# Attention, routed experts and feed-forward on one core: logits' units respaced, buffers moved by 160 bytes, a longer last filler

## The chip, the cores and the metric

The kernel runs on one core of a Trainium2 chip. The metric is the device time of one execution in microseconds (us). A profile of one execution by the hardware profiler shows what each engine did: TensorE (PE, its weight loads apart as PEld), VectorE (DVE), ScalarE (ACT), GpSimd (POOL) and SyncE (SP, which here only issues DMAs).

## The reference

Three blocks in a row, all in float32. Attention: 4 batches x 8 heads, 576 tokens, head size 64; scores below the row's maximum minus `tau` are masked out before the softmax. The result is rearranged to 2304 tokens x 512 features. Then a mixture of 8 experts: each token goes to the expert with the largest cosine similarity (the logits), through `relu(x @ w1[e]) @ w2[e]`, weighted by the softmax probability of that expert. Then a gated feed-forward with 1536 hidden features.

```python
    scores = np.where(scores >= thresh, scores, -1000000000.0)
    ...
    logits = xn @ en.T / tau
    expert_idx = np.argmax(logits, axis=1)
    ...
        h = np.maximum(x[mask] @ w1[e], 0.0)
        out[mask] = gate_w[mask, None] * (h @ w2[e])
    ...
    g = x @ w_gate
    silu = g * (1.0 / (1.0 + np.exp(-g)))
    val = x @ w_val
    return (silu * val @ w_out).astype(np.float32)
```

## The kernel before

Large products are made from operands split in two fp32r parts, `hi` and `lo`, with three matmuls in place of one.

**Attention** (`attention`, L166) works on 16 pairs of heads with 9 score tiles each, 144 steps, numbered g = 0 to 143. A step of TensorE is a turn of one loop (from L390): values of the step two back (`values`, L354, ten 128x66 matmuls in the trace, where the program has five float32 ones), scores of the step two ahead (`scores_tile`, L311), transposes of this step's probabilities (`probs_t`, L335). Between scores and transposes VectorE takes the maximum (L545), ScalarE the exponential (L416), VectorE the mask (`prob`, L557); after the transposes ScalarE copies them out of PSUM (`prob_t`, L423). Three PSUM buffers go round for scores and transposes, two for the values.

**Logits' units.** The logits of tokens whose heads are all done are computed among the attention steps. A unit takes some (token tile, feature chunk) blocks: `tokens_t` (L343) transposes them from `x_sb` in place of a step's probabilities, ScalarE copies them out, `logits` (L371) multiplies them with the expert embeddings (128x8 matmuls), ScalarE copies the sums out (`logits_out`, L441). A unit has its own place in the list UNITS, which sets the order on TensorE, ScalarE and VectorE: `unit_order` (L143) puts it behind the step that the table `logit_units` (L126) names. A unit has no scores, so in the turn two ahead of it TensorE has none to compute. Tiles 0 to 8 need heads of the first eight pairs (`s_x` at 8, counted by GpSimd's `normalise`, L662), tiles 9 to 17 those of the second eight; the latter are summed in parts (`part`) and added at the end by VectorE (L634 to L638).

**Experts** (`experts`, L783): after a routing stage, tokens are gathered slot by slot (128 rows, L102), transposed (`rows_t`, L908), multiplied with w1 (`hidden`, L916, L927: hp) and w2 (`output`, L943, L954: yp). Stationary operands are slices of `xt` and `ht`, moving operands are 512 columns of the weights. `keep_warm` (L959) issues matmuls whose result nobody reads, at three places of the routing stage; both operands are taken from the start of the same weight chunk. WARM (L780) has their numbers.

**Feed-forward** (`feed_forward`, L1210): 6 groups of 384 tokens by 12 chunks of 128 hidden features, 72 steps. A step has 24 matmuls of 384 columns (`gate_value`, L1331: gp and vp, stationary the weights, moving `f_xt`) and 9 of 512 columns (`add_out`, L1345: op, stationary `st`, moving the weights).

**Buffers.** The weights, `x_sb` and what lies beside them are placed from the top of SBUF downwards (`Weights`). The other buffers are placed upwards from the bottom, in the order of the code; those of the three stages begin behind `norm` (in `build`, L1489) and take each other's place. 

Of the kernel before, what the change touches and what calls it, by code (L numbers as in the profile page):

```python
# [7 lines left out]
F32 = mybir.dt.float32  # L8
F32R = mybir.dt.float32r
I32 = mybir.dt.int32  # L10
ALU = mybir.AluOpType
# [11 lines left out]
KC = FEAT // 128  # L23
# [89 lines left out]
TILES = 9  # L113
# [8 lines left out]
STEP, LOGITS = "step", "logits"  # L122
# [3 lines left out]
def logit_units():  # L126

    units = [(((t, t + 1), range(KC)), (10 + t // 3, 1 + 3 * (t % 3))) for t in range(TILES)]  # L130
    units += [(((TILES + 2 * n, min(TILES + 2 * n + 2, 2 * TILES)), range(0, 2)), (13 + n // 3, 1 + 3 * (n % 3)))
              for n in range(5)]
    thirds = ((0, 4), (4, 8), (8, 9))
    units += [(((TILES + a, TILES + b), range(2, 3)), (15, 1 + 3 * n)) for n, (a, b) in enumerate(thirds)]
    units += [(((TILES + a, TILES + b), range(3, 4)), None) for a, b in ((0, 4), (5, 9), (4, 5))]
    return units


LOGIT_UNITS = logit_units()
HEADS_4_5 = TILES + 7  # L140


def unit_order():  # L143

    behind = {at: n for n, (_, at) in enumerate(LOGIT_UNITS) if at}
    order = []
    for g in range(STEPS):
        order.append((STEP, g))
        if (g // TILES, g % TILES) in behind:
            order.append((LOGITS, behind[g // TILES, g % TILES]))  # L150
    return order + [(LOGITS, n) for n, (_, at) in enumerate(LOGIT_UNITS) if not at]


UNITS = unit_order()
UNIT_OF = {what: u for u, what in enumerate(UNITS)}

# [9 lines left out]
def attention(nc, q, k, v, tau, emb, moe_tau, w1, w2, x_rows, ys_dram, weights, ident, consts, logit,  # L166
# [7 lines left out]
    with ExitStack() as ctx:  # L174
        def sb(name, shape, dt=F32):
            return ctx.enter_context(nc.sbuf_tensor(name, shape, dt))

        def sem(name):
            return ctx.enter_context(nc.semaphore(name))
# [23 lines left out]
        part = sb("part", [128, 3, TILES, EXPERTS])  # L203
# [39 lines left out]
        s_part = sem("s_part")  # L243
# [167 lines left out]
        def _(act):  # L411
# [29 lines left out]
            def logits_out(u, n):  # L441
                (first, end), chunks = LOGIT_UNITS[n][0]
                act.wait_ge(s_o, u + 1)
                if first < TILES:
                    dst = logit[:, first:end, :]
                else:
                    dst = part[:, max(0, chunks[-1] - 1), first - TILES:end - TILES, :]
                nc.scalar.activation(dst.rearrange("p t e -> p (t e)"), o_ps[u % 2][:, 0:EXPERTS * (end - first)],
                                     ACT.Copy).then_inc(s_o_sb, 1)

# [55 lines left out]
            for u in range(len(UNITS) + 1):  # L506
                if u < len(UNITS):
                    what, g = UNITS[u]
# [5 lines left out]
                if u + 2 < len(UNITS):  # L514
                    what, g = UNITS[u + 2]
                    if what == STEP:
                        exp_tile(u + 2, g)
                if u >= 1:
                    what, g = UNITS[u - 1]
                    if what == STEP and g < LAST:  # L520
                        values_out(u - 1, g)
                    elif what == STEP:
                        last_values_out(u - 1, g)
                    else:
                        logits_out(u - 1, g)
                if u < len(UNITS) and UNITS[u][0] == STEP:
                    p, t = UNITS[u][1] // TILES, UNITS[u][1] % TILES
# [11 lines left out]
        def _(dve):  # L539
            V = nc.vector  # L540
# [29 lines left out]
            def last_sum_inv(g):  # L570
                t, u = g - LAST, UNIT_OF[STEP, g]
                dve.wait_ge(s_o, behind(g))
                if t == 0:
                    dve.wait_ge(s_x, PAIRS - 2)
                if t < 8:
                    last = V.tensor_scalar(row_sum[:, 1, t:t + 1], o_ps[u % 2][:, D:D + 1], 1e-9, None, ALU.add)
                else:
                    for side in range(2):
                        rows = slice(TAIL * side, TAIL * (side + 1))
                        last = V.tensor_scalar(row_sum[rows, 1, t:t + 1],  # L580
                                               o_ps[u % 2][rows, V_COLS * side + D:V_COLS * side + D + 1],
                                               1e-9, None, ALU.add)
                last.then_inc(s_last_inv, 1)
                dve.wait_ge(s_last_inv, 2 * t + 1)
                V.reciprocal(row_inv[:, 1, t:t + 1], row_sum[:, 1, t:t + 1]).then_inc(s_last_inv, 1)
# [36 lines left out]
            for u in range(behind(STEPS - 1) + 2):  # L622
                what, g = UNITS[u + 1]
                if what == STEP:
                    max_tile(u + 1, g)
                what, g = UNITS[u]
# [4 lines left out]
                what, g = UNITS[u - 2]  # L631
                if u >= 2 and what == STEP and g >= LAST:
                    last_sum_inv(g)
            dve.wait_ge(s_o_sb, UNIT_OF[LOGITS, HEADS_4_5] + 1)  # L634
            V.tensor_tensor(part[:, 0, :, :], part[:, 0, :, :], part[:, 1, :, :], ALU.add).then_inc(s_part, 1)
            dve.wait_ge(s_part, 1)
            dve.wait_ge(s_o_sb, len(UNITS))
            V.tensor_tensor(logit[:, TILES:2 * TILES, :], part[:, 0, :, :], part[:, 2, :, :], ALU.add)  # L638
# [138 lines left out]
        self.inv = ctx.enter_context(nc.psum_tensor("inv", [128, 2, SLOTS], F32))  # L777


WARM = (6, 20, 14)  # L780


def experts(nc, slot_rows, ys_dram, w1, w2, wg, wv, wo, weights, slot_tab, ident, logit, best, norm, squares, gate,  # L783
# [5 lines left out]
    with ExitStack() as ctx:  # L789
# [117 lines left out]
        def _(pe):  # L907
            def rows_t(i, buf, arrived):  # L908
                pe.wait_ge(s_x[buf], arrived)

                for c in range(KC):
                    last = nc.tensor.transpose(xb[:, 128 * c:128 * (c + 1)], x_in[:, buf, 128 * c:128 * (c + 1)],
                                               ident[:])
                last.then_inc(s_xt, 1)
# [44 lines left out]
            def keep_warm(n):  # L959
                w = weights.ring[0][:, 0, 0, :]  # L960
                for _ in range(n):
                    nc.tensor.matmul(yp[:], w[:, 0:128], w[:, 0:PSUM_BANK], start=True, stop=True)

            keep_warm(WARM[0])
            pe.wait_ge(s_pad, 1)
# [5 lines left out]
            last.then_inc(s_rank, 1)  # L971
            keep_warm(WARM[1])
            pe.wait_ge(s_row, 1)
            for t in range(T):
                last = nc.tensor.matmul(r.inv[:], r.row_b[:, t, :], r.token_b[:, t, :, :], start=(t == 0), stop=(t == T - 1))
            last.then_inc(s_inv, 1)
            keep_warm(WARM[2])
            rows_t(0, 0, 16)
# [493 lines left out]
def spread(a, n=128):  # L1472
    return a.rearrange("(a b) -> a b", a=1).broadcast_to([n, 1])


def build(nc, q, k, v, tau, emb, moe_tau, w1, w2, w_gate, w_val, w_out, out):
    x_rows = nc.dram_tensor("x_rows", (TOKENS, FEAT), F32, kind="Internal").ap()
    ys = nc.dram_tensor("ys", (SLOTS * 128, FEAT), F32, kind="Internal").ap()
    with ExitStack() as ctx:
        ident = ctx.enter_context(nc.sbuf_tensor("ident", [128, 128], F32))  # L1480
        pos = ctx.enter_context(nc.sbuf_tensor("pos", [128, TOK_TILES], I32))
        gate = ctx.enter_context(nc.sbuf_tensor("gate", [128, TOK_TILES], F32))
        token_of = ctx.enter_context(nc.sbuf_tensor("token_of", [128, SLOTS], I32))
        slot_tab = ctx.enter_context(nc.sbuf_tensor("slot_tab", [1, 5, SLOTS + 1], I32))
        weights = Weights(nc, ctx)
        logit = ctx.enter_context(nc.sbuf_tensor("logit", [128, TOK_TILES, EXPERTS], F32))
        best = ctx.enter_context(nc.sbuf_tensor("best", [128, TOK_TILES], F32))
        squares = ctx.enter_context(nc.sbuf_tensor("squares", [128, TOK_TILES], F32))
        norm = ctx.enter_context(nc.sbuf_tensor("norm", [128, TOK_TILES], F32))  # L1489
        s_xrows = ctx.enter_context(nc.semaphore("r_xrows"))  # L1490
        s_filled = ctx.enter_context(nc.semaphore("r_filled"))
        consts = Consts(nc, weights)
        attention(nc, q, k, v, spread(tau), emb, spread(moe_tau), w1, w2, x_rows, ys, weights, ident, consts, logit,
                  squares, s_xrows, s_filled)
        with ExitStack() as rows_ctx:
            slot_rows = SlotRows(nc, rows_ctx, x_rows, token_of)
            experts(nc, slot_rows, ys, w1, w2, w_gate, w_val, w_out, weights, slot_tab, ident, logit, best, norm, squares,
                    gate, s_filled, consts, s_xrows, pos, token_of)
        feed_forward(nc, ys, out, w_gate, w_val, w_out, weights, pos, gate, ident)
# [47 lines left out]
```

## Time and profile before

| | us |
|---|---|
| median of 3 runs | 1186.64 (1180.28 to 1188.91) |
| profiled execution | 1188.04 |
| its span, first to last instruction | 1186.1 |
| TensorE busy | 1122.5 (95%) |
| VectorE busy | 546.3 (46%) |
| ScalarE busy | 508.2 (43%) |
| GpSimd busy | 245.5 (21%) |

Attention lasts to about 393 us of the span, routing to about 412, the experts to about 687, the feed-forward to the end. The granted TensorE clock is a mean 0.982 of full speed (2.4 GHz); 0.5 is the lower of its two levels, 1.2 GHz. Matmuls are pipelined: a matmul's duration is longer than the distance to the next one's start, and a row of several (x14) lasts from the first one's start to the last one's end. In brackets stands an engine's idle time before a row, with what ended it.

### The profile page before, as it was taken

The numbers are of one execution on the slowest core, as the hardware profiler recorded it, in microseconds if no ns is written. First come the engines' busy times: TensorE is split into PE (matmuls) and PEld (weight loads), VectorE is DVE, ScalarE is ACT, GpSimd is POOL, SyncE is SP. The second block draws the span as 40 slices with busy tenths as digits, with TensorE's granted clock in tenths as the row PEclk, the third lists the DMA queues.
The fourth block names the chain that finished last, engine by engine and source line by source line (L and its number), as shares of the span: only waits on it lengthen the run. The fifth ranks groups of instructions, "written<-read, shape, count | busy, mean of one in ns | idle before, by whom it ended". The sixth has DMA issues, their size and how long they took to land. (4 is left out here: it accounts for less than half of the span.)

```text
span 1186.1 us, 19312 instructions
## 1 busy us (share of the span) xinstructions
PE 1122.5 (95%) x6837; PEld 1029.8 (87%) x6838; DVE 546.3 (46%) x910; ACT 508.2 (43%) x900; POOL 245.5 (21%) x185
## 2 busy tenths in 40 slices
PE   5999999999999799999999929999999999999996
PEld 4999999999999578888888829999999999999996
DVE  4777777765566455555433524322322323223221
ACT  4777777778676454444442423121221221212211
POOL 1433445442520101111111111212030030200000
PEclk9999999999999899999999969999999999999999
DMA  4222332341101645465424331001010010000000
GB/s 161 70 83 100 132 102 96 119 180 55 55 2 60 206 160 178 140 232 180 152 101 160 112 114 62 27 25 30 1 54 1 1 53 0 27 0 0 28 1 27
DMA packets 35687, 97.36 MB, mean 82 GB/s; under 512 B 2968, under 2 KB 5272, under 8 KB 35616
## 3 DMA queue, kind: packets, MB, share of 16 engines
q1 hardware_dynamic: 28880, 74.88, 18.1%
q0 software_dynamic: 6560, 21.50, 5.4%
q8 instruction: 46, 0.75, 0.3%
q14 instruction: 25, 0.20, 0.1%
q10 hardware_dynamic: 176, 0.02, 0.0%
HBM read 79.61 MB, written 16.78 MB: 81 GB/s over the span
## 5 line engine op out<-in xcount | busy, mean ns | idle before, releaser
L367 PE MATMUL o_ps<-v_in,prob_t 128*128 128x66 f32 (+1 forms) x1440 | 181.2, 274 | 0.2 <-ACT prob_t L423 0.2
L367 PEld LDWEIGHTS o_ps<-v_in,prob_t 128*128 128x128 f32 x1440 | 175.8, 195 | 0.4 <-ACT prob_t L423 0.4
L1440 DVE TENSOR_TENSOR act_in<-gp,sig 128x384 f32<-128x384 f32 x72 | 40.1, 557 | 277.4 <-ACT sig L1386 277.4
L545 DVE TENSOR_REDUCE neg_max<-scores 128x1 f32<-128x576 f32 x144 | 109.0, 757 | 108.5 <-PE scores L330 108.2
L1386 ACT ACTIVATE sig<-gp 128x384 f32<-128x384 f32 x72 | 35.4, 491 | 281.1 <-PE vp L1331 281.1
L423 ACT ACTIVATE prob_t<-scores 128x640 f32<-128x640 f32 (+3 forms) x164 | 112.9, 689 | 91.8 <-PE scores L340 84.9
L557 DVE SCALAR_TENSOR_TENSOR prob<-scores,thresh,expo 128x576 f32<-128x576 f32 x144 | 116.5, 809 | 3.1 <-ACT expo L416 3.1
L340 PE MATMUL scores<-ident,prob 128*128 128x128 f32 x720 | 105.8, 279 | 8.6 <-DVE prob L557 8.6
L330 PE MATMUL scores<-kt_hi,qt 128*128 128x288 f32 x320 | 104.3, 342 | 5.7 <-DVE kt_lo L617 3.0
L416 ACT ACTIVATE expo<-scores,neg_max 128x576 f32<-128x576 f32 x144 | 107.1, 744 | 4.0 <-DVE neg_max L545 4.0
L1331 PE MATMUL gp<-f_xt_hi,w_hi 128*128 128x384 f32 x288 | 99.8, 347 | 1.4 <-DVE f_xt_lo L1429 1.4
L1331 PE MATMUL gp<-f_xt_hi,w_lo 128*128 128x384 f32 x288 | 98.1, 341 | 0.0
L1331 PE MATMUL gp<-f_xt_lo,w_hi 128*128 128x384 f32 x288 | 98.1, 340 | 0.0
L1331 PE MATMUL vp<-f_xt_hi,w_hi 128*128 128x384 f32 x288 | 97.5, 339 | 0.0
L1331 PE MATMUL vp<-f_xt_lo,w_hi 128*128 128x384 f32 x288 | 97.5, 339 | 0.0
L1331 PE MATMUL vp<-f_xt_hi,w_lo 128*128 128x384 f32 x288 | 97.4, 338 | 0.0
L1304 POOL DMA_INDIRECT out<-stage,out_row x18 | 17.6, 979 | 384.3 <-ACT stage L1399 381.0
L340 PEld LDWEIGHTS scores<-ident,prob 128*128 128x128 f32 x720 | 86.7, 143 | 11.0 <-DVE prob L557 10.9
L330 PE MATMUL scores<-kt_lo,qt 128*128 128x288 f32 x320 | 91.5, 302 | 0.0
L1345 PE MATMUL op<-w_hi,st_hi 128*128 128x512 f32 x216 | 85.8, 397 | 1.7 <-DVE st_lo L1446 1.7
L1345 PE MATMUL op<-w_lo,st_hi 128*128 128x512 f32 x216 | 86.1, 398 | 0.0
L1345 PE MATMUL op<-w_hi,st_lo 128*128 128x512 f32 x216 | 85.1, 394 | 0.0
(201 smaller groups left out, 2134.4 us busy)
## 6 DMA issues: line engine op xcount, KB each, us to landing
stage<-in_moe_w SPq DMA_DIRECT2D x18, 1024.0 KB, 5.4
stage_more<-in_moe_w SPq DMA_DIRECT2D x14, 1024.0 KB, 7.6
q_raw<-in_q SPq DMA_DIRECT2D x16, 640.0 KB, 5.1
k_raw<-in_k SPq DMA_DIRECT2D x16, 576.0 KB, 3.8
ys<-y_out POOLq DMA_DIRECT2D x21, 256.0 KB, 2.3
v_in<-in_v SPq DMA_DIRECT2D x16, 330.0 KB, 2.9
stage<-in_moe_w_val SPq DMA_DIRECT2D x3, 1024.0 KB, 5.7
x_rows<-x_sb SPq DMA_DIRECT2D x1, 2304.0 KB, 9.1
```

The costliest lines, as they stand in the source:

```text
L330: last = nc.tensor.matmul(scores[u % 3][:, half, 0:HALF], qt[:, par, c:c + 128], kt[:, par, keys], start=(m == 0 and kt is kt_hi), stop=(m ...
L340: last = nc.tensor.transpose(dst[:, 128 * c:128 * (c + 1)], prob[:, g % 3, key:key + 128], ident[:])
L367: last = nc.tensor.matmul(dst, prob_t[:, u % 3, 128 * c:128 * (c + 1)], src, start=(c == 0), stop=(c == KEY_CHUNKS - 1))
L416: nc.scalar.activation(expo[:, g % 3, :].rearrange("p (a c) -> p a c", a=2), scores[u % 3][:, :, 0:HALF], ACT.Exp, bias=neg_max[:, g % TIL ...
L423: nc.scalar.activation(prob_t[:, u % 3, 0:cols], scores[u % 3][:].rearrange("p a c -> p (a c)")[:, 0:cols], ACT.Copy).then_inc(s_pt_sb, 1)
L545: V.tensor_reduce(neg_max[:, t:t + 1], scores[u % 3][:, :, 0:HALF], mybir.AxisListType.XY, ALU.max, negate=True).then_inc(s_max, 1)
L557: V.scalar_tensor_tensor(prob[:, g % 3, :].rearrange("p (a c) -> p a c", a=2), scores[u % 3][:, :, 0:HALF], thresh[:, t:t + 1], expo[:, g ...
L1304: nc.gpsimd.indirect_dma_start(out=out, out_offset=bass.IndirectOffsetOnAxis(ap=out_row[:, n:n + 1], axis=0), in_=y[:, t, :], in_offset=No ...
L1331: last = nc.tensor.matmul(dst[:, 0:GT], w[a][:, 3 * (f // 4) + which, k, 128 * (f % 4):128 * (f % 4 + 1)], xt[buf][b][:, k, :], start=(n = ...
L1345: last = nc.tensor.matmul(op[t][:], st[a][:, f % 2, 128 * t:128 * (t + 1)], w[b][:, 3 * (f // 4) + 2, f % 4, :], start=(f == 0 and n == 0) ...
L1386: nc.scalar.activation(sig[:], gp[f % 2][:, 0:GT], ACT.Sigmoid).then_inc(s_sig, 1)
L1440: nc.vector.tensor_tensor(act_in[:], gp[f % 2][:, 0:GT], sig[:], ALU.mult).then_inc(s_c, 1)
```

## The change

Four edits, shown below.

- The units get other places, and the table names the step g itself. Tiles 0 to 8 stand behind steps 79, 83, ... 111 (before: 91, 94, ... 115), four pairs of tiles with two chunks behind 116, 120, 124, 128 (before five units behind 118, 121, ... 130, the fifth with one tile). The last token tile has one unit with three chunks behind 133, and two units with four tiles follow behind 137 and 141 (before 136, 139, 142 with 4, 4 and 1 tiles). The three units behind the last step are as before. 17 units among the steps become 16; the blocks are the same 72.
- `logits_out` and VectorE's addition follow: the last tile's three chunks are summed by the unit itself, so the addition of the second part leaves that tile out.
- WARM's last number goes from 14 to 22.
- An unused buffer is placed ahead of all buffers of the three stages, so that the first of them starts a multiple of 512 bytes from the weights. In the built program it has 160 bytes: `kt_hi`, `x_in` and `rows` move from 18752 to 18912, and all that follows them moves by the same 160. `x_sb` starts at 192480.

```diff
-    units = [(((t, t + 1), range(KC)), (10 + t // 3, 1 + 3 * (t % 3))) for t in range(TILES)]
...
-    thirds = ((0, 4), (4, 8), (8, 9))
-    units += [(((TILES + a, TILES + b), range(2, 3)), (15, 1 + 3 * n)) for n, (a, b) in enumerate(thirds)]
+    units = [(((t, t + 1), range(KC)), 79 + 4 * t) for t in range(TILES)]
+    units += [(((TILES + 2 * n, TILES + 2 * n + 2), range(0, 2)), 116 + 4 * n) for n in range(4)]
+    units += [(((2 * TILES - 1, 2 * TILES), range(0, 3)), 133)]
+    units += [(((TILES + a, TILES + a + 4), range(2, 3)), 137 + a) for a in (0, 4)]
...
-HEADS_4_5 = TILES + 7
+HEADS_4_5 = TILES + 6
...
-        if (g // TILES, g % TILES) in behind:
-            order.append((LOGITS, behind[g // TILES, g % TILES]))
+        if g in behind:
+            order.append((LOGITS, behind[g]))
...
-                    dst = part[:, max(0, chunks[-1] - 1), first - TILES:end - TILES, :]
+                    dst = part[:, chunks[-1] - 1 if len(chunks) == 1 else 0, first - TILES:end - TILES, :]
...
-            V.tensor_tensor(part[:, 0, :, :], part[:, 0, :, :], part[:, 1, :, :], ALU.add).then_inc(s_part, 1)
+            rest = TILES - 1
+            V.tensor_tensor(part[:, 0, 0:rest, :], part[:, 0, 0:rest, :], part[:, 1, 0:rest, :], ALU.add).then_inc(s_part, 1)
...
-WARM = (6, 20, 14)
+WARM = (6, 20, 22)
...
+        here = -(-nc.sbuf_base // 32) * 32
+        ctx.enter_context(nc.sbuf_tensor("to_weights", [128, (weights.x_start - here) % 512 // 4], F32))
```

The order on TensorE, before, from the transposes of the second unit's tokens (`scores<-ident,x_sb`) to the values behind its logits (`o_ps<-emb_t,prob_t`); the next unit stands three tiles further:

```order
L351 MATMUL scores<-ident,x_sb 128x128 x4
L367 MATMUL o_ps<-v_in,prob_t 128x66 x5
L330 MATMUL scores<-kt_hi,qt 128x288
L330 MATMUL scores<-kt_lo,qt 128x288
L330 MATMUL scores<-kt_hi,qt 128x288
L330 MATMUL scores<-kt_lo,qt 128x288
L340 MATMUL scores<-ident,prob 128x128 x5
L379 MATMUL o_ps<-emb_t,prob_t 128x8 x4
L340 MATMUL scores<-ident,prob 128x128 x5
L367 MATMUL o_ps<-v_in,prob_t 128x66 x5
```

Here no scores stand between the logits and the next transposes of probabilities. The same place with the change (the lines' numbers are one lower there):

```order
L350 MATMUL scores<-ident,x_sb 128x128 x4
L366 MATMUL o_ps<-v_in,prob_t 128x66 x5
...
L339 MATMUL scores<-ident,prob 128x128 x5
L378 MATMUL o_ps<-emb_t,prob_t 128x8 x4
L329 MATMUL scores<-kt_hi,qt 128x288
L329 MATMUL scores<-kt_lo,qt 128x288
L329 MATMUL scores<-kt_hi,qt 128x288
L329 MATMUL scores<-kt_lo,qt 128x288
L339 MATMUL scores<-ident,prob 128x128 x5
L366 MATMUL o_ps<-v_in,prob_t 128x66 x5
L339 MATMUL scores<-ident,prob 128x128 x5
L366 MATMUL o_ps<-v_in,prob_t 128x66 x5
```

The logits are now followed by scores; the turn without scores comes one later and holds values.

## Rows read from the trace of the kernel before

**Rows 1.** Busy time by stretch: us; five engines busy (instructions); clock; DMA share; GB/s.

```profile
253.90:280.50 26.60, 25.02 (x214) 24.61 (x212) 15.84 (x30) 20.91 (x43) 7.98 (x5) 1.00 0.19 61
321.50:325.00 3.50, 3.50 (x16) 3.48 (x17) 0.97 (x2) 2.35 (x4) 2.08 (x1) 0.51 0.00 0
...
430.00:680.00 250.00, 249.51 (x1193) 203.76 (x1192) 122.20 (x122) 109.10 (x130) 37.80 (x40) 1.00 0.48 167
```

**Rows 2.** Timeline of TensorE, logits three tiles ahead of a unit: start, us, what.

```profile
238.46 0.96 PE L379 MATMUL o_ps<-emb_t,prob_t 128*128 128x8 f32 x8
239.90 0.76 PE L340 MATMUL scores<-ident,prob 128*128 128x128 f32 x5 [0.49 <-DVE prob L557]
```

**Rows 3.** Timeline of TensorE, two turns ahead of the first unit.

```profile
229.94 1.23 PE L367 MATMUL o_ps<-v_in,prob_t 128*128 128x66 f32 x10
231.38 0.77 PE L340 MATMUL scores<-ident,prob 128*128 128x128 f32 x5 [0.21 <-DVE prob L557]
```

**Rows 4.** Timeline of TensorE, a turn of values and a half-sized unit's logits.

```profile
350.83 1.23 PE L367 MATMUL o_ps<-v_in,prob_t 128*128 128x66 f32 x10
351.87 0.38 PE L330 MATMUL scores<-kt_hi,qt 128*128 128x288 f32 x1
...
355.07 0.51 PE L379 MATMUL o_ps<-emb_t,prob_t 128*128 128x8 f32 x4
356.03 0.40 PE L330 MATMUL scores<-kt_hi,qt 128*128 128x288 f32 x1 [0.45 <-ACT prob_t L423]
```

**Rows 5.** Timeline of GpSimd and TensorE at steps 79 to 81.

```profile
202.79 1.16 POOL L666 TENSOR_TENSOR x_sb<-o_sb,row_inv 128x576 f32<-128x576 f32 x1
...
206.26 0.71 PE L340 MATMUL scores<-ident,prob 128*128 128x128 f32 x5
```

**Rows 6.** Timeline of TensorE from the last filler to the second slot's first product.

```profile
404.74 3.44 PE L962 MATMUL yp<-w_hi 128*128 128x512 f32 x14
410.08 0.99 PE L912 MATMUL xb<-ident,x_in 128*128 128x128 f32 x4 [1.89 <-DMA x_in<-x_rows,token_of]
412.75 1.21 PE L927 MATMUL hp<-w_hi,xt_hi 128*128 x2 [1.68 <-DVE xt_lo L1083]
...
420.42 0.60 PE L912 MATMUL xb<-ident,x_in 128*128 128x128 f32 x4
...
422.91 0.73 PE L927 MATMUL hp<-w_hi,xt_hi 128*128 x2 [0.55 <-DVE xt_lo L1083]
...
428.63 0.60 PE L912 MATMUL xb<-ident,x_in 128*128 128x128 f32 x4
```

**Rows 7.** Busy time by stretch around the last filler, columns as in rows 1.

```profile
402.00:404.20 2.20, 0.00 (x0) 0.00 (x0) 2.17 (x5) 0.00 (x0) 0.00 (x0) 1.00 1.03 387
...
412.70:414.00 1.30, 1.25 (x3) 1.07 (x4) 0.00 (x0) 0.00 (x0) 0.00 (x0) 0.50 0.72 199
```

**Rows 8.** Timeline of TensorE, part of the second filler.

```profile
397.88 3.56 PE L962 MATMUL yp<-w_hi 128*128 128x512 f32 x15
```

**Rows 9.** Timeline of TensorE, an expert's second product: second and last of 24.

```profile
505.31 0.39 PE L954 MATMUL yp<-w_lo,ht_hi 128*128 x1
...
510.45 0.39 PE L954 MATMUL yp<-w_hi,ht_lo 128*128 x1
```

**Rows 10.** Timeline of TensorE, one step of the feed-forward: first gp, first op, next gp.

```profile
1046.26 0.34 PE L1331 MATMUL gp<-f_xt_hi,w_hi 128*128 128x384 f32 x1
...
1050.50 0.40 PE L1345 MATMUL op<-w_hi,st_hi 128*128 128x512 f32 x1
...
1052.61 0.34 PE L1331 MATMUL gp<-f_xt_hi,w_hi 128*128 128x384 f32 x1
```

**Rows 11.** Groups by line: number, busy, mean ns of one, idle before.

```profile
L1331 PE MATMUL gp<-f_xt_hi,w_hi 128*128 128x384 f32 x288 | 99.8, 347 | 1.4 <-DVE f_xt_lo L1429 1.4
...
L954 PE MATMUL yp<-w_hi,ht_hi 128*128 x168 | 68.3, 407 | 0.5 <-DVE ht_lo L1093 0.5
...
L927 PE MATMUL hp<-w_hi,xt_hi 128*128 x176 | 58.4, 413 | 2.2 <-DVE xt_lo L1083 2.2
```

More of the change, by code:

```diff
@@ L126, in logit_units @@
 def logit_units():
-    units = [(((t, t + 1), range(KC)), (10 + t // 3, 1 + 3 * (t % 3))) for t in range(TILES)]
-    units += [(((TILES + 2 * n, min(TILES + 2 * n + 2, 2 * TILES)), range(0, 2)), (13 + n // 3, 1 + 3 * (n % 3)))
-              for n in range(5)]
-    thirds = ((0, 4), (4, 8), (8, 9))
-    units += [(((TILES + a, TILES + b), range(2, 3)), (15, 1 + 3 * n)) for n, (a, b) in enumerate(thirds)]
+    units = [(((t, t + 1), range(KC)), 79 + 4 * t) for t in range(TILES)]
+    units += [(((TILES + 2 * n, TILES + 2 * n + 2), range(0, 2)), 116 + 4 * n) for n in range(4)]
+    units += [(((2 * TILES - 1, 2 * TILES), range(0, 3)), 133)]
+    units += [(((TILES + a, TILES + a + 4), range(2, 3)), 137 + a) for a in (0, 4)]
     units += [(((TILES + a, TILES + b), range(3, 4)), None) for a, b in ((0, 4), (5, 9), (4, 5))]
```

## The prediction

> **What bounds the kernel now.** I read the windows by stage first. In one pair of the attention part that carries logits' units, TensorE is busy 25.02 of 26.60 us; in the experts it is busy 249.51 of 250.00 us [rows 1]. So the end is set by TensorE's own stream: a term counts if it shortens TensorE's work, or a wait of TensorE. Then I read the timeline of TensorE at the places that the change touches, for two things: where it stands idle, and the pace, that is, the time from one matmul's start to the next one's (a matmul's own duration overlaps its neighbour's and is no price).
>
> All sums below are made against the profiled execution, 1188.04 us; the median of the runs shown is 1186.64, so 1.4 us comes off at the end. One per cent, about 12 us, is what I take a measurement of this kernel to tell from no change.
>
> **Part 1: the units' spacing.** TensorE's program has, in the turn two before a unit, no score tile to compute. Where units are three tiles apart, that turn is also the one that holds the previous unit's logits. There eight logits matmuls start at 238.46 and the transposes of the next tile only at 239.90: 1.44 us, 0.49 of it marked idle, waiting for VectorE's prob [rows 2]. Before the first unit of all, the turn without scores holds ten value matmuls instead, and takes 229.94 to 231.38: again 1.44, with 0.21 idle [rows 3]. So VectorE's chain sets 1.44 whatever TensorE has to put in it. With four tiles between, the values stand in that turn and the logits in one that has scores. A values turn with scores takes 1.04 (350.83 to 351.87). A logits turn with scores takes 0.96, and not less, since the scores wait for ScalarE's copy: in the half-sized unit at 355.07 the scores start at 356.03 after 0.45 idle [rows 4]. Per unit that was 1.44 + 1.04 = 2.48 and becomes 0.96 + 1.44 = 2.40: 0.08 us. The old table has 15 units that follow another by three tiles: 15 x 0.08 = 1.2 us. The idle rows alone would give 15 x (0.49 - 0.21) = 4.2 us, which is the far end, because the new wait behind the logits takes back the rest.
>
> The unit that is saved takes a turn without scores with it, 1.44 - 1.04 = 0.40, and the 0.45 idle behind the half-sized logits, of which about 0.2 stays with the new unit of three blocks: 0.6 us. The blocks transposed and multiplied are the same 72, so nothing else leaves TensorE. **Spacing: -1.8 us, between 0 and -4.2.** What could eat it: the first unit now stands behind tile 79 and needs the eighth normalised head. GpSimd has it at 202.79 + 1.16 = 203.95; the unit's transposes would come at 206.26 [rows 5], 2.3 us later, so that wait stays empty. Should it not, the cover is those 2.3 us and the cost what exceeds them, once. VectorE's shorter addition of the partial logits (8 tiles for 9) and ScalarE's one copy fewer lie beside TensorE's work and cost nothing.
>
> One stretch of the old units also lost clock: the granted clock is 0.51 in 321.50 to 325.00, the 1.2 GHz level, with TensorE busy in all of its 3.50 us, while a pair with the same three units has 1.00 [rows 1]. At half clock that stretch can have cost up to 1.75 us. It stands among the idle places that the new spacing shortens, but the clock can fall elsewhere; I take half: **-0.8, between 0 and -1.75.**
>
> **Part 2: the filler.** The last filler ends at 404.74 + 3.44 = 408.18, the first rows' transposes start at 410.08 when the gathered rows land, and the first product at 412.75 [rows 6]. From 412.70 on the clock is 0.50 [rows 7]. That product takes 412.75 to 420.42 = 7.67 us; the next, warm, 422.91 to 428.63 = 5.72: 1.95 us lost, and 0.39 more in the four transposes (0.99 against 0.60) [rows 6]. Eight more fillers at 0.226 us (below) are 1.81 us, so they end at 409.99, 0.09 us before the rows are there. If they overran, TensorE would be late by a few tenths. A gap of 1.7 us before the product stays. A stretch of 2.2 us without any matmul, right behind a dense one, kept the clock at 1.00 [rows 7]. I take most of the loss as saved: **-2.0, between +0.2 and -2.3.**
>
> **Part 3: the pad.** It moves every buffer behind it by 160 bytes, so that xt, ht, f_xt and st, which were 352 bytes past a multiple of 512 from the weights, stand on one. No instruction comes or goes. The question is whether TensorE's pace depends on how its two operands lie to each other. One stream shows it: the filler, whose stationary and moving operand start at the same address. Fifteen of them take 3.56 us, so (3.56 - 0.39) / 14 = 0.2264 us each [rows 8]. The experts' products move the same 512 columns, but with the stationary operand 352 bytes off: 505.31 to 510.45 is 22 paces, 0.2336 [rows 9]. In the feed-forward, 24 products of 384 columns take 1046.26 to 1050.50, 0.1767 each, and the nine of 512 take 2.11, 0.2344 each; the step of 6.35 us holds nothing else [rows 10]. Both operands are fp32r and other engines are busy in all three, so the address relation is the difference I see.
>
> If the pad gives all of them the filler's pace: 512 columns gain 0.0072 in the experts (3 x 176 + 3 x 168 = 1032 matmuls [rows 11]: 7.4 us) and 0.0080 in the feed-forward (288 / 4 = 72 steps x 9 = 648: 5.2 us). For 384 columns no aligned row exists; by the same ratio, 0.2264 / 0.2340, 0.1767 becomes 0.1710, and 6 x 288 = 1728 [rows 11] gain 9.9 us. Together **-22.5 us**. The ends are 0 (the filler is quick for another reason, such as loading the same weights again) and, as nothing excludes a loss, +22.5 (the new relation is as much worse as the old is above the filler). I take -22.5, because the filler is the nearest row in size, type and clock.
>
> The Trainium skill ("SBUF — State Buffer", section "Who interferes with whom") speaks against this part: TensorE has two independent read ports, one for the moving operand and one for the weight load, and PE never waits on anyone. By that rule the pad is worth nothing and the sum is the first rival's. No run here shows the ports by themselves; the 0.0072 us a matmul between filler and expert [rows 8, 9] speak against the rule.
>
> The keys in attention move too; their slices then lie 0, 128, 256 and 384 bytes off multiples of 512 and the queries 256 off, so they meet the same relation only in a quarter of the products; values and transposes are limited by weight loads. I take 0 there.
>
> **Sum:** -22.5 - 1.8 - 0.8 - 2.0 = -27.1; 1188.0 - 27.1 = 1160.9, and 1.4 less against the runs: about **1160 us**.
>
> **Rivals.**
> - *The addresses don't matter.* For it: the pace scales with columns (0.2336 / 512 and 0.1767 / 384 are both 0.46 ns a column [rows 9, 10]), as a plain limit of streaming would; only 15 fillers speak otherwise. Then -4.6 remains: 1186.6 - 4.6 = **1182** (1178 to 1187). Chance 0.35.
> - *Only part of it:* the 512-column products gain and those of 384 don't, or half of each: 22.5 becomes about 12: **1170**. Chance 0.08.
> - *Slower.* The two reads of TensorE now meet in the same place of the memory on every matmul. The price is the mirror, +22.5 - 4.6: **1204**. It decides from a pace of 0.239 at 512 columns upwards (5 ns on 3408 matmuls is 17 us, which eats the 4.6 and one per cent). Against it: the filler has this relation and is the quickest stream of all. Chance 0.05.
> - *The change doesn't do what it says:* in the built program x_sb starts at 192480 and the first padded buffer at 18912, 339 x 512 apart, so it does.
>
> My forecast has 0.52, with a range of its own of 1153 to 1167. **Range** over the cases: 1152 to 1185; the mirror and the outer parts of the others are left out, under 0.2. Faster by over 1% (below 1175): 0.52 and most of "part", 0.58. Within 1%: the first rival and a little, 0.36. Slower: 0.06.
>
> **What would show it.** Part 3: the pace of yp and hp falls from 0.234 to about 0.227, a step of the feed-forward from 6.35 to 6.15 us; if it stays at 6.35, this part is wrong and with it the forecast. Part 1: no idle of 0.49 behind logits; instead 0.21 behind values, and no long wait of the transposes behind tile 79. Part 2: clock 1.00 through the first rows, first product 5.7 us long. If the clock falls a little later instead, part 2 gives under one microsecond.

## The result, and the profile after

The changed kernel takes 1178.45 us (median of 15 runs), the kernel before, beside it, 1186.48. The ratio, which is formed from all runs and not from the two medians, is 0.9946, 95% interval 0.9926 to 0.9965, that is 6.4 us less (4.2 to 8.8). The time lies inside the range, but under one per cent, and the gain of 6.4 us is about a quarter of the 27 forecast.

The profiled execution of the change takes 1178.48 us, its span is 1176.5, the mean granted clock 0.983. By stage, from the starts and ends of TensorE's rows in both traces:

| stage | before, us | after, us | difference | forecast |
|---|---|---|---|---|
| start to first filler (attention) | 393.39 | 398.09 | +4.70 | -2.6 |
| first filler to second slot's first product | 29.52 | 27.52 | -2.00 | -2.0 |
| from there to the last yp | 263.49 | 258.53 | -4.96 | -7.4 |
| last yp to the 13th gp | 29.87 | 28.23 | -1.64 | 0 |
| 13th gp to the last op | 461.54 | 455.80 | -5.74 | -15.1 |

The 13th matmul of gp is taken as a mark because the first twelve run partly at the lower clock, which lasts 23.9 us before (until 714.0 us) and 20.5 after (until 707.0). The filler's stage has the number forecast, the pad's two stages gave 10.7 us in place of 22.5, and attention lost where it should have gained.

Windows of the change, columns as in rows 1; the last one answers to the experts' stretch of [rows 1]:

```profile
304.20:307.70 3.50, 3.50 (x17) 3.50 (x17) 0.72 (x1) 1.51 (x3) 3.23 (x1) 0.51 0.52 210
331.50:338.40 6.90, 6.90 (x35) 6.89 (x34) 1.68 (x3) 2.49 (x5) 0.00 (x0) 0.51 0.00 0
...
430.00:680.00 250.00, 249.23 (x1217) 207.12 (x1217) 125.80 (x125) 111.50 (x135) 39.64 (x40) 1.00 0.48 167
```

The experts fit more matmuls into the same 250 us (1217 records for 1193). But in attention there are now 10.2 us at the lower clock, where the kernel before had 3.4.

TensorE's timeline where units stand four tiles apart, which answers to [rows 2, 3]:

```profile
233.37 0.96 PE L378 MATMUL o_ps<-emb_t,prob_t 128*128 128x8 f32 x8
234.32 0.40 PE L329 MATMUL scores<-kt_hi,qt 128*128 128x288 f32 x1
...
235.51 1.23 PE L366 MATMUL o_ps<-v_in,prob_t 128*128 128x66 f32 x10
236.95 0.77 PE L339 MATMUL scores<-ident,prob 128*128 128x128 f32 x5 [0.21 <-DVE prob L556]
```

The two turns take 0.95 and 1.44 = 2.39 us; 2.40 was forecast, with 0.21 idle behind the values.

Where attention lost its time: TensorE, VectorE and GpSimd of the change around step 111's unit, each from its own timeline.

```profile
301.81 0.29 PE L329 MATMUL scores<-kt_lo,qt 128*128 128x288 f32 x1
303.34 0.77 PE L339 MATMUL scores<-ident,prob 128*128 128x128 f32 x5 [1.24 <-DVE prob L556]
303.94 1.97 PE L366 MATMUL o_ps<-v_in,prob_t 128*128 128x66 f32 x10
...
298.57 0.81 DVE L556 SCALAR_TENSOR_TENSOR prob<-scores,thresh,expo 128x576 f32<-128x576 f32 x1
299.29 2.16 DVE L562 TENSOR_SCALAR row_sum<-o_sb 128x9 f32<-128x9 f32 x1
...
302.48 0.81 DVE L556 SCALAR_TENSOR_TENSOR prob<-scores,thresh,expo 128x576 f32<-128x576 f32 x1
...
298.79 2.64 POOL L659 TENSOR_TENSOR kt_lo<-k_raw,kt_hi 128x1152 fp32r<-128x1152 f32 x1 [14.31 <-ACT k_raw L473]
```

Read upwards: TensorE waits 1.24 us for VectorE's prob; that is late because the row sums before it, 128 x 9 numbers, take 2.16 us. They end at 301.45, when GpSimd's `kt_lo` ends (298.79 + 2.64 = 301.43). Right after TensorE's wait the granted clock falls to 0.51, the first window above. The same happens at step 120's unit: row sums of 2.17 us at 326.73 under `kt_lo` at 326.23, a wait of 1.24, and 6.8 us at the lower clock. The other thirteen row sums take 0.16. In the kernel before all fifteen do, and none starts less than 1.9 us ahead of a `kt_lo`; in the pair that holds step 111 it is 2.5 us:

```profile
293.86 0.16 DVE L563 TENSOR_SCALAR row_sum<-o_sb 128x9 f32<-128x9 f32 x1
...
296.38 2.63 POOL L659 TENSOR_TENSOR kt_lo<-k_raw,kt_hi 128x1152 fp32r<-128x1152 f32 x1 [13.79 <-ACT k_raw L474]
```

The row sums stand behind the mask of tile 4 (`g % TILES == 4`), and a unit behind tile 3 now comes ahead of them.

For the paces, four yp rows of an expert (second, tenth, sixteenth, last of 24) and one step of the feed-forward, which answer to [rows 9, 10]:

```profile
506.62 0.40 PE L954 MATMUL yp<-w_lo,ht_hi 128*128 x1
...
508.47 0.39 PE L954 MATMUL yp<-w_hi,ht_hi 128*128 x1
...
509.83 0.39 PE L954 MATMUL yp<-w_hi,ht_hi 128*128 x1
...
511.64 0.39 PE L954 MATMUL yp<-w_hi,ht_lo 128*128 x1
...
1038.27 0.33 PE L1331 MATMUL gp<-f_xt_hi,w_hi 128*128 128x384 f32 x1
...
1042.45 0.39 PE L1345 MATMUL op<-w_hi,st_hi 128*128 128x512 f32 x1
...
1044.53 0.33 PE L1331 MATMUL gp<-f_xt_hi,w_hi 128*128 128x384 f32 x1
```

The mean over 22 yp paces is (511.64 - 506.62) / 22 = 0.2282 us, from 0.2336. From the second to the tenth they take 0.2313 each, over the last eight 0.2263, the filler's pace. So the short step is there, but a stream reaches it only after some nine matmuls, and each transpose, wait or change of shape starts the next stream anew. The medians of hp's steps at full clock show it: with the change, after the first, 233, 236, 224, 231, 236, 228, 232, 231 ns and then 227 to the end of the 24; in the kernel before they go round 232, 238, 237, 231, 234, 235, 233 to the end and never settle. In the feed-forward the 24 products take 0.1742 each (0.1767 before), the nine of 512 take 0.2311 (0.2344), and a step 6.26 us (6.35).

The filler's place, which answers to [rows 6]:

```profile
408.29 5.26 PE L962 MATMUL yp<-w_hi 128*128 128x512 f32 x22
413.60 0.66 PE L912 MATMUL xb<-ident,x_in 128*128 128x128 f32 x4
415.93 0.73 PE L927 MATMUL hp<-w_hi,xt_hi 128*128 x2 [1.68 <-DVE xt_lo L1083]
...
425.61 0.72 PE L927 MATMUL hp<-w_hi,xt_hi 128*128 x2 [0.55 <-DVE xt_lo L1083]
```

The fillers end at 413.55 and the rows' transposes follow at once. The clock still falls, later and for less long: 0.50 from 416.9 to 420.3, inside the first product, which takes 7.19 us instead of 7.67. Of the stage's 2.00 us, 1.15 lie ahead of the last filler (393.39 to 404.74 before, 398.09 to 408.29 after): there the clock was at its lower level from 393.2 to 396.6 before and is not now.

### The profile page after: what moved, and what is told of

It reads as the page before. It is cut to its first block and busy times, and to the rows that moved or that the text cites. A ratio compares the mean times of both kernels' runs of the same rounds, so it can differ in the third digit from the quotient of the medians.

```text
span 1176.5 us, 19323 instructions
## 1 busy us (share of the span) xinstructions
PE 1115.8 (95%) x6845; PEld 1027.3 (87%) x6846; DVE 549.5 (47%) x910; ACT 507.2 (43%) x898; POOL 246.7 (21%) x185
```

## The experiments

Times in us; a ratio is to the kernel before in the same series, with its 95% interval. Single runs of the kernel before lie between 1176.44 and 1192.30, so stages are compared in the traces and totals by their intervals. Two things in attention differ from trace to trace without any change to it. One is the first pair of heads (from its first `neg_max` to the next pair's), 19.4 to 26.9 us: the scores start 0.24 us apart at first and 0.13 later, and this turns at about 30 us in the kernel before and at 19 in a run with everything 128 bytes lower (below). The other is where the clock falls: a pair with three units takes 26.55 us at full clock and 28.14 with one fall. So attention is best compared from the second pair on:

| trace | first pair | second pair to first filler | falls of the clock inside |
|---|---|---|---|
| before | 25.08 | 353.70 | 1 |
| the filler alone (attention as before) | 26.88 | 352.10 | 0 |
| the pad alone (units as before) | 21.44 | 355.18 | 2 |
| the change | 25.06 | 358.59 | 2 |
| row sums behind tile 3 | 25.26 | 351.36 | 0 |
| the spacing alone, row sums behind tile 3 | 25.27 | 351.40 | 0 |

Falls that begin in the last 1.2 us, at the first filler, are not counted; they change the stretch by under 0.1 us.

**The three parts alone.** The pad alone (the two lines of `to_weights` added to the kernel before):

> The kernel before with the pad alone (spacing and filler as they were). Theory: the pad is worth about 10.7 us of the 1186.5 (5.0 in the experts' hp and yp, 5.7 in the feed-forward), since long streams fall into a step of 226.7 ns for 512 columns and 173.3 ns for 384: 1175.8 us, within 2.5; yp's matmuls go from 234 to 227-229 ns, and the attention ends (first filler) at 393.4, as before. Rival 1, addresses do not matter and the pace seen in the changed kernel belongs to the clock or the spacing: 1186.5 us, yp 234 ns. Rival 2, the pad moves buffers of the attention and is what delayed it there: first filler 3 us or more later than 393.4, and about 1180 us.

Measured: 1174.90, ratio 0.9912 (0.9886 to 0.9938): -10.4 us. Second slot to last yp 258.50, 13th gp to last op 455.80, as in the change. All fifteen row sums take 0.16; the first filler is at 391.36, and attention from the second pair on is 1.5 us longer than before, which is one more fall of the clock (28.13 us for 26.55 in that pair). The first theory holds, both rivals fall.

The change without the pad (the same two lines taken out):

> The changed kernel without the pad (spacing and filler as in the change). Theory: the spacing costs the attention 4.7 us and the filler gives back 2, so 1189 us within 2.5; yp at 234 ns; first filler at 398 us, with two row sums of over 2 us on VectorE behind GpSimd's kt_lo in pairs 12 and 13. Rival 1 (addresses do not matter): like the changed kernel, 1178.5. Rival 2 (the pad delayed the attention): first filler at 391 to 393 us, 1182 us, row sums of 0.16 us.

Measured: 1190.32, ratio 1.0034 (1.0014 to 1.0053): +4.0 us. First filler at 398.07, row sums of 2.16 us at 299.37 and 326.72. The rest of the change is slower than the kernel before. -10.4 and +4.0 make -6.4, as the whole has; their intervals reach 3.1 and 2.3 us to either side.

The filler alone:

```diff
-WARM = (6, 20, 14)
+WARM = (6, 20, 22)
```

> The kernel before with the longer last filler alone. Theory: first filler to second hp goes from 29.5 to 27.5 us as in the changed kernel, 1184.5 us. Rival: the drop of the granted clock only moves to a later place, and the time stays at 1186.5 us within 0.7.

Measured: 1183.73, ratio 0.9990 (0.9975 to 1.0005): -1.2 us, not told from nothing. In its trace first filler to second product is 27.26 us, 2.3 less than before, and the first slot's product runs at clock 1.00. But the pad alone, with the old 14 fillers, shows the same: 27.00 us, and a first product of 5.56 us, the full clock's:

```profile
410.36 0.72 PE L927 MATMUL hp<-w_hi,xt_hi 128*128 x2 [1.68 <-DVE xt_lo L1083]
...
415.92 0.60 PE L912 MATMUL xb<-ident,x_in 128*128 128x128 f32 x4
```

And the run with the row sums behind tile 3 (below) has 22 fillers, yet takes 29.00 us there, with the clock at 0.50 from 410.5 to 413.9 and a first product of 7.18. Over all eighteen traces the clock falls in the first rows or their product in three of four with 14 fillers and in six of fourteen with 22; in three more of these it falls during the last filler instead. So one trace of either kind does not show what the filler gives.

**The collision.** The change with the row sums a tile earlier:

```diff
-                    if g >= TILES and g % TILES == 4:
+                    if g >= TILES and g % TILES == 3:
```

> The changed kernel with VectorE's row sums of each pair a tile earlier (behind the mask of tile 3 instead of tile 4 of the next pair). Theory: the two row sums of 2.16 us were stopped by GpSimd's kt_lo (2.64 us), which then no longer overlaps them: all fifteen take 0.16 us, no wait of TensorE over 1 us in pairs 12 and 13, the granted clock stays at 1.0 there, first filler at about 391 us and 1171.5 us (1170 to 1174). Rival 1, ScalarE is late behind a unit at tile 3 and VectorE's row sum is a bystander: the waits of 1.2 to 1.5 us stay, 1178.5 us. Rival 2, the collision moves to other pairs, where a unit now lies before tile 3: as many long row sums at other places, 1176 to 1180 us.

Measured: 1167.21, ratio 0.9857 (0.9830 to 0.9885), a little under the 1170 to 1174 expected. All fifteen row sums take 0.160 to 0.166 us; the two places where the clock fell:

```profile
304.20:307.70 3.50, 3.29 (x30) 3.15 (x28) 2.37 (x4) 1.64 (x5) 3.50 (x2) 1.00 0.59 238
331.50:338.40 6.90, 6.90 (x61) 6.81 (x60) 4.78 (x9) 4.82 (x11) 4.17 (x2) 1.00 0.01 2
```

First filler at 391.12, 7.0 us earlier than in the change. Pairs 12 and 13, counted from 0 (from one first `neg_max` to the next), take 24.43 and 24.39 for 27.43 and 28.65.

The change with another form of the row sums, at their old place:

```diff
-                V.tensor_scalar(row_sum[:, p % 2, :], ..., 1e-9, None, ALU.add)
+                V.tensor_reduce(row_sum[:, p % 2, :], ..., mybir.AxisListType.X, ALU.add)
```

> The changed kernel with VectorE's fifteen row sums formed by a reduction over an axis of one element in place of the addition of a constant to it (the 1e-9 that is added to each row sum is left out); they stay behind tile 4. Theory: VectorE was stopped by what this form of operation needs of a port that it shares with GpSimd, and a reduction does not need it: all fifteen take 0.1 to 0.3 us even while kt_lo runs on GpSimd, no wait of TensorE over 1 us in pairs 12 and 13, 1171 us (1168 to 1174). Rival 1 (any operation of VectorE that reads o_sb waits for GpSimd, or the time comes from what follows it): two of 2.16 us stay and 1178.5 us. Rival 2 (the reduction itself is slow, or the reciprocal behind it is stopped instead): the reciprocal takes 2 us at the two places and the time stays.

Measured: 1171.50, ratio 0.9895 (0.9860 to 0.9929). VectorE, then GpSimd, at the first of the two places:

```profile
297.74 0.16 DVE L562 TENSOR_REDUCE row_sum<-o_sb 128x9 f32<-128x9 f32 x1
297.94 0.21 DVE L567 RECIPROCAL row_inv<-row_sum 128x9 f32<-128x9 f32 x1
...
297.24 2.64 POOL L659 TENSOR_TENSOR kt_lo<-k_raw,kt_hi 128x1152 fp32r<-128x1152 f32 x1 [14.31 <-ACT k_raw L473]
```

The reduction lies inside `kt_lo` and takes 0.16. (The 1e-9 is left out in this kernel.) It is the form of the operation that meets GpSimd, not VectorE's work as such; in the change's own trace a mask, the maxima and `thresh`, a `tensor_scalar` too but over one number, run under `kt_lo` in 0.82, 0.76 and 0.21 us, as elsewhere. The Trainium skill ("SBUF — State Buffer", section "Who interferes with whom") has this as a lock on a port pair that VectorE and GpSimd share: copies and `tensor_scalar` may take it in their fast modes, `tensor_reduce` never, and who comes second is fully blocked. 2.16 us ending with `kt_lo`, against 0.16, agrees.

The collision put into the kernel before, with the row sums behind tile 5:

```diff
-                    if g >= TILES and g % TILES == 4:
+                    if g >= TILES and g % TILES == 5:
```

> The kernel before (its own spacing, filler and addresses) with the row sums a tile later, behind the mask of tile 5, which puts them where kt_lo runs on GpSimd in pairs 1 to 14. Theory: fourteen of the fifteen row sums take about 2.1 us, TensorE waits 1.2 to 1.5 us behind each, and the attention is 14 x 1.2 = 17 us (without any fall of the clock) to 14 x 3.4 = 48 us (with one each, as in the changed kernel) longer: 1202 to 1232 us. Rival (the collision is harmless in itself, and it was the unit behind tile 3 that left TensorE without work): long row sums, but the time within 3 us of 1184.5.

Measured: 1196.15, ratio 1.0103 (1.0073 to 1.0134): +12 us, under the range expected. Nine row sums collide, not fourteen; from pair 10 on the units delay the row sums by 4.1 us and `kt_lo` by only 1.3, so that they start 0.6 us after its end. VectorE, GpSimd and TensorE in pair 1:

```profile
53.33 2.17 DVE L563 TENSOR_SCALAR row_sum<-o_sb 128x9 f32<-128x9 f32 x1
...
52.83 2.64 POOL L659 TENSOR_TENSOR kt_lo<-k_raw,kt_hi 128x1152 fp32r<-128x1152 f32 x1 [11.17 <-ACT k_raw L474]
...
57.39 0.77 PE L340 MATMUL scores<-ident,prob 128*128 128x128 f32 x5 [0.54 <-DVE prob L557]
```

Without a unit beside it TensorE waits 0.54 us, a pair takes 21.57 for 20.81, and the clock stays at 1.00. So the collision alone costs 0.76 us a pair; with a unit's turn without scores behind it the wait is 1.24 and the clock falls too, which makes 3.0 and 4.3 us a pair. The fall does not follow every time: eight traces have the collision at both places, and at the second the clock fell in all of them, at the first in five. In the other three (256 and 128, all 128 lower, f_xt at 352) the same wait there costs 1.4 us: the pair takes 25.84 to 25.87 for 24.43. The profiled run was the quickest of the four here (1191.25); its nine collisions make 6.8 us, and where the rest of the 12 us lies, no trace shows.

The two units one step later (111 to 112, 120 to 121), row sums as in the change:

> The changed kernel with the two units behind tile 3 (steps 111 and 120) one step later, behind tile 4; row sums stay behind tile 4, addresses as in the change. Theory: the row sums then come before the unit, 2.5 us ahead of kt_lo as at the other places: fifteen of 0.16 us and 1169 us (1166 to 1173). Rival (any two units in the last pairs do this, whatever their tile): long row sums or waits over 1 us stay, 1176 us or more.

Measured: 1171.86, ratio 0.9880 (0.9846 to 0.9913); fifteen row sums of 0.16 us, at the first place 298.03 with `kt_lo` at 300.55. So it matters behind which tile the unit stands, and not that there is a unit in these pairs.

The spacing alone, without the collision (the change's units, row sums behind tile 3, filler and addresses as before):

> The spacing alone (filler and addresses as before) with the row sums behind tile 3, so that they meet no kt_lo. Theory: what the first part of the prediction forecast for the spacing holds once the collision is gone: 1.8 us less, with 1.7 us more where the fall of the clock at 321.5 us goes: 1181 to 1183 us, no clock at half speed before 380 us. Rival (the rest of the gain of the kernel with all three parts comes from something else than the spacing): 1185 us within 1.

Measured: 1182.99, ratio 0.9981 (0.9957 to 1.0005): -2.3 us, by its interval not told from nothing, nor from the rival. The trace says more. First filler at 391.11, 2.3 earlier than before, no lower clock until 390.0. From the second pair on it is 351.40 for 353.70, and 1.60 of these 2.30 are the fall of the clock that the kernel before has and the filler alone, with the same attention, has not (352.10). The spacing itself gives 0.70. A full unit adds as much to its pair as it did: (26.55 - 20.91) / 3 = 1.88 us at three tiles, (24.66 - 20.91) / 2 = 1.88 at four, and 1.92 in the next pair.

**The distances.** Unused buffers before xt, ht, f_xt and st in the change put each at a chosen distance; for the first run:

```diff
+        sb("off_xt", [128, 64])
         xt = [sb(f"xt_{p}", [128, FEAT], F32R) for p in ("hi", "lo")]
```

> The changed kernel with the row operands put off the multiple of 512 bytes again: the experts' xt and the feed-forward's f_xt 256 bytes past it, the experts' ht and the feed-forward's st 128 bytes past it. The weights stay where they are. Theory (the distance of the two operands modulo 512 sets the step): all four lose the step of 226.7 and 173.3 ns, hp, yp near 234 ns, gp and vp near 176.7. Rival 1 (the pattern repeats every 256 bytes): hp at 227 to 229 and vp at 173.3 as in the changed kernel, yp near 234. Rival 2 (every 128 bytes): all four as in the changed kernel.

> As the run with 256 and 128 bytes, but xt and f_xt 64 bytes past the multiple, ht and st 32 bytes past it. Theory: all four at the slower steps, near 234 and 176.7 ns, since no distance but 0 gives the short one. Rival 1 (the pattern repeats every 64 bytes): hp and vp at 227 to 229 and 173.3, yp near 234. Rival 2 (only distances near 352, as in the kernel before, are bad): all four as in the changed kernel, hp 228.7, yp 228.9, vp 173.3 ns.

> The changed kernel with everything, weights and row operands, 128 bytes lower, so that the distances of the operands stay multiples of 512 and the absolute addresses change. Theory (only the distance counts): hp, yp at 227 to 229 ns, vp at 173.3, 1178.5 us. Rival (the absolute address counts, and the pad hit a good one by luck): hp, yp near 234, vp near 176.7, about 1189 us.

> The changed kernel with xt 128, ht 256, f_xt 32 and st 352 bytes past the multiple of 512. From the two runs before: hp and yp have the short step at distances 0 and 256 alone, so hp should be at 232 to 234 ns here and yp at 228 to 229. The feed-forward: theory, f_xt repeats every 64 bytes, so 32 acts as 352 did: vp 176.7 ns; rival, only 352 was bad: vp 173.3. op: theory, st's own distance sets it: 236 ns at 352, as in the kernel before; rival, f_xt's or nothing: 232.

> The changed kernel with f_xt 96 bytes past the multiple of 512, st on it, xt 32 and ht 64 past it. Theory from the experts: the step repeats every 256 bytes, so 96 does in the feed-forward what 352 did before: vp 176.7 ns, and op 236 if it follows f_xt. Rival: only 352 itself is bad, vp 173.3 to 174. hp and yp: 233 to 234 ns, as 32 and 64 gave.

> The changed kernel with f_xt alone of the feed-forward's buffers back at 352 bytes past the multiple of 512 as in the kernel before (st on it), xt 416 and ht 0. Theory: f_xt's distance sets gp and vp, and st's nothing: vp 176.7 ns; op 232 if it is not f_xt's either, 236 if the products before it set its start. Rival: f_xt's distance does nothing and something else of the kernel before did: vp 173.3. hp near 233 ns, yp at 228 to 229.

Measured: mean ns from a matmul's start to the next of the same product, at full clock, gaps of 300 ns and more left out (the first step of each stream of hp and yp, 302 to 340 ns in every run, and three waits in op); in brackets the bytes of the row operand past a multiple of 512.

| run | hp (xt) | yp (ht) | gp, vp (f_xt) | op (st) |
|---|---|---|---|---|
| before | 234.2 (352) | 233.8 (352) | 178.4, 176.6 (352) | 234.3 (352) |
| the change | 228.4 (0) | 228.4 (0) | 177.0, 173.3 (0) | 231.2 (0) |
| 256 and 128 | 228.4 (256) | 232.3 (128) | 177.3, 173.3 (256) | 232.2 (128) |
| 64 and 32 | 233.4 (64) | 233.3 (32) | 175.0, 173.3 (64) | 232.8 (32) |
| all 128 lower | 227.2 (0) | 227.6 (0) | 177.2, 173.3 (0) | 231.2 (0) |
| swapped | 232.4 (128) | 228.2 (256) | 175.4, 173.6 (32) | 234.4 (352) |
| f_xt at 96 | 233.0 (32) | 233.2 (64) | 178.5, 176.6 (96) | 230.8 (0) |
| f_xt at 352 | 233.5 (416) | 228.3 (0) | 178.4, 176.6 (352) | 231.0 (0) |

Those eight rows say four things. With everything moved together the short step stays: the distance counts, not the address. hp and yp have it at 0 and 256 and at no other of the distances tried, so the theory of a multiple of 512 falls to the rival of 256. gp and vp, where the row operand is the moving one, have it at 0, 32, 64 and 256, and lose it at 96 and 352, which are the same modulo 256; gp's mean differs among the good ones, 175.0 to 177.3. And op goes from 231 to 234 with st's distance, behind either kind of vp. Missed by the first theories: vp kept 173.3 to 173.6 at 256, 64 and 32, where 176.7 was expected, and op is 234.4 at 352 for 236.

**The best put together.** First, row sums behind tile 3 with everything 128 bytes lower; then the same with f_xt at 64 bytes:

> The changed kernel with row sums behind tile 3 and everything 128 bytes lower: the two best of the runs put together. Theory: the sum of what each gave, 1167 less 1.0 in the experts: 1166 us (1164 to 1172), no row sum over 0.2 us. Rival: yp's shorter mean step in the run with everything 128 lower was chance: as with the row sums alone, 1167 to 1171.

Measured: 1171.56, ratio 0.9891 (0.9867 to 0.9915), so no quicker than the row sums alone, as the rival had it; hp and yp do keep 227.1 and 227.6 ns.

> The kernel with everything 128 bytes lower and the row sums behind tile 3, with f_xt 64 bytes past the multiple of 512 and st on it. From the single runs: gp 175.0 ns (64 bytes) in place of 177.2, vp 173.3, op 231.2 (st at 0): a step of the feed-forward 12 x 2.2 = 26 ns shorter, 72 of them 1.9 us. Theory: the distances of the two operands act one by one and add up: first gp to op's end 1.9 us shorter, 1165 to 1170 us. Rival: gp's shorter step came with st's distance, and goes with it: gp 177, nothing gained.

Measured: 1166.13, ratio 0.9837 (0.9808 to 0.9866), 19 us (16 to 23) under the kernel before, its interval below that of the change but overlapping that of the row sums alone (0.9830 to 0.9885). gp 175.1, vp 173.3 and op 228.2 ns: op gained where nothing was expected. One step of its feed-forward:

```profile
1037.00 0.34 PE L1333 MATMUL gp<-f_xt_hi,w_hi 128*128 128x384 f32 x1
...
1041.16 0.39 PE L1347 MATMUL op<-w_hi,st_hi 128*128 128x512 f32 x1
...
1043.22 0.34 PE L1333 MATMUL gp<-f_xt_hi,w_hi 128*128 128x384 f32 x1
```

6.22 us for 6.26 in the change; 13th gp to last op 452.42, from 455.96 with f_xt at 0: 3.5 us where 1.9 was expected. So the distances do not act one by one: op's step with st at 0 is 231 behind f_xt at 0 and 228 behind f_xt at 64. The medians of op's eight steps show how: 229, 233, 236, 224, 231, 236, 228, 232 ns in the change, which never settles in so short a stream, and 229, 232, 231 and then 227 here.

## Why the prediction was wrong

**Part 3, the pad: right in kind, the term too large.** "If the pad gives all of them the filler's pace" was the step that failed. It gives that pace, 0.2263, at the end of a stream of 24, while the steps up to the tenth matmul take 0.2313. Per product, from the table: hp gained 5.8 ns x 528 = 3.1 us and yp 5.4 x 504 = 2.7, where 7.4 was forecast; op 3.1 x 648 = 2.0 for 5.2; gp 1.4 x 864 = 1.2 and vp 3.3 x 864 = 2.9, where 9.9 was taken "by the same ratio" from a row of another shape. 11.9 in all; the two stages show 10.7, the pad alone 10.4 (7.3 to 13.5). The likeliest case was the full price, and what happened is the rival called "only part", which had 12 us and a chance of 0.08. A row in hand spoke against it: the fifteen in [rows 8] are the last of a filler of 20, past its slow start, while the last filler's fourteen in [rows 6], same operands and full clock, take (3.44 - 0.39) / 13 = 0.2346 each from the first one on. Its first step alone is 0.312; the other twelve take 0.229 each, close to what yp then took (0.2282).

**The first rival** (addresses don't matter) falls by the pad alone, and with it the rule of the Trainium skill ("SBUF — State Buffer", section "Who interferes with whom") that PE's two read ports are independent and PE waits on no one, as far as it is read as saying that operands' places are free: 234.2 against 228.4 ns with the same instructions. That the two reads meet in the memory is one way to explain it; no run shows the ports themselves.

**Part 1, the spacing: two terms missed, and the cover named was the wrong one.** 2.39 us for the two turns came out as the 2.40 forecast, but no unit became cheaper by it: about 1.9 us before and after. Without the collision the spacing gives 0.70 us in place of 1.8, about what the saved unit alone was to give (0.6); what takes back the 0.08 a unit is open. The fall of the clock gives 1.60 in place of 0.8, where the kernel before happens to have it: the old spacing shows none, one and two falls in the three traces without a collision. That the two make 2.3 for 2.6 is luck. And under "what could eat it" stood only the wait for the eighth head, which indeed stayed empty. The step that failed is that VectorE's other work was taken to lie beside TensorE's as before: a unit behind tile 3 moved the row sums from 2.5 us ahead of GpSimd's `kt_lo` to 0.5 behind its start, the form of operation blocks, and after a wait of 1.24 us of TensorE the clock was at its lower level for 3.4 and 6.8 us. The price was 7.2 us (358.59 and 351.36 from the second pair on), which turned a gain into +4.7.

**Part 2, the filler: the number came out, by luck.** -2.0 us for -2.0 in its stage, but 1.15 of them lie ahead of the longer filler, where the clock did not fall this time. "If the clock falls a little later instead" came true: the first product lost 1.6 us (7.19 against 5.56 at full clock with the pad) in place of 1.95. The filler alone gives -1.2 us (-3.0 to +0.6), so its worth is not shown.

**The slower mirror** is excluded: no product became slower.

## What to carry to other kernels

A pace read from one stream is its mean at that length: look whether the steps inside it are even, and price short streams by their own first steps. When a step is moved on one engine, list what it passes on the other engines too, small operations included, and look which long operation of GpSimd each of VectorE's then falls under. Where TensorE is full, price a new wait with the clock: here 1.2 us of waiting cost 1.4 us where the clock stayed up and 3.0 and 4.3 where it fell. And where a stage comes out as forecast, look in its rows whether the part that was changed is the part that gained.

## What the hardware showed that was not expected

- TensorE's step from matmul to matmul depends on the distance of its two operands, and 0 and 256 bytes act alike, as do 96 and 352: 227.2 to 228.4 against 232 to 234 ns at 512 columns, 173.3 against 176.6 at 384. Which distances are good differs between the products: 32 and 64 bytes were good for gp and vp, bad for hp and yp. A sign (moving minus stationary operand) would join the two lists; no run tests that.
- A `tensor_scalar` over 128 x 9 numbers took 2.16 us under a `tensor_tensor` of GpSimd and ended with it; one over 128 x 1 numbers took 0.21 as always, and a reduction over the same 128 x 9 took 0.16.
- hp's mean step is 227.2 with all buffers 128 bytes lower and 228.4 without, at equal distances: its stream is at 227 from the fourth step on (232, 231, 227) in place of the tenth. What decides how soon a stream settles is open.
